# Attention into two expert layers on one core: key input loaded in stripes, with TensorE kept running at the start, and rows scattered by halves

## The chip, the cores and the metric

One core of one Trainium2 chip. The metric is the device time of one execution in microseconds (us), lower is better; most executions of one kernel agree within 0.3%.

## What is computed

Attention over pooled keys, then two mixture-of-experts layers of which each row takes one expert.

```python
B, N, C = q.shape                      # 2, 12288, 128
kv_pool = kv.reshape(B, H//4, 4, W//4, 4, C).mean(axis=(2, 4))   # H 384, W 32
k = v = kv_pool.reshape(B, -1, C) @ w_sr                         # 768 keys a batch
s = (q @ k.transpose(0, 2, 1)) / np.sqrt(C)
a = np.exp(s - s.max(-1, keepdims=True)); a /= a.sum(-1, keepdims=True) + 1e-9
x = (a @ v).reshape(B * N, D)
# layer 1 and layer 2 (8 experts, hidden width 1024), e = argmax of x @ w_gate:
out[mask] = gate_w[mask, None] * (np.maximum(x[mask] @ w1[e], 0) @ w2[e])
# layer 2 multiplies by sigmoid(x @ w_output_gate)[:, e] as well
```

## The kernel before

The queries come in 96 blocks of 256 rows (`NBLK`), four blocks to an iteration and two to a group of 512 rows. Each engine has a program of its own, in an order written out by hand; semaphores tie them together.

**Keys.** Of each batch, 768 keys are six chunks of 128. `load_kv` (L658) brings a chunk with four DMAs of 256 KB: partition p holds the 4x4 pixels of key p, and each DMA fetches one of the four image rows, 2 KB a partition. For the first batch VectorE adds the 16 pixels in one reduction (`kv_sum`, L1474), TensorE turns the result (L1040), ScalarE scales it (L1318), TensorE multiplies by `w_sr` (L1044, L1045), ScalarE and VectorE split the product into a high and a low part (`kv_high` L1323, `kv_low` L1480). For the second batch GpSimd adds in four steps (L884) in place, and TensorE turns and projects a chunk in two steps inside `turn_q` (L1058 for the turn, L1062 and L1063 for the projection) of blocks 4 to 15, a chunk every two blocks.

**Blocks.** `turn_q` (L1066) turns the queries of block c, four blocks ahead; `score` (L1079) multiplies them by all keys in three products; VectorE takes the maximum (L1503), ScalarE the exponential (L1349), TensorE turns the probabilities (L1103), multiplies them by the values (L1119) and by the gate matrix (`turn_rows`, L1138). ScalarE writes those rows to `rows` (L1373), two buffers that the groups use in turn. The lead (`lead`) fills this pipeline before the loop: `turn_q` of blocks 0 to 3 and `score` of blocks 0 and 1.

**Queries.** Each group of queries is one DMA of 256 KB on SyncE's queue (L647) into one of two buffers. Group 2 (blocks 4 and 5) and group 3 (blocks 6 and 7) are issued at the head of the first iteration, behind all key loads of both batches and the first four raw weight loads (L678, L683).

**Scatter.** When the places of a group's rows are known (`place`, L362), GpSimd issues four indirect DMAs (L390), 128 rows each, to the expert's bucket in HBM. In the loop of the queries it then splits expert weights (L903, L905). A buffer of `rows` may be written again when all four DMAs of its group have landed: ScalarE waits for that in `rows_out` (L1373), VectorE in `tile_rows_out` (L1632) of layer 1, whose rows go to `y_bucket` in the same way. The tiles of both layers are 256 rows; `up` is L1203, `down` L1220, the rows' gate product L1235. A tile's expert weights come from `w_table` in loads of 1 MB.

The waits that the change touches:

```python
# load_kv, L657        sp.wait_ge(kv_summed, c + 1)            second batch
# turn_q, L1057        pe.wait_ge(kv_fold, FOLDS * (late - KC + 1))
# rows_out, L1372      wait(act, r1.scattered[g], i, 64, 64 * (c // 4))
# tile_rows_out, L1624 if c % 2 == 0: wait(dve, r2.scattered[g], i, 64, 64 * (c // 4))
```

## Time and profile before

| | |
|---|---|
| median of 3 runs (lowest, highest) | 1969.69 us (1968.4, 1975.17) |
| profiled execution, its own time | 1974.21 us |
| its span | 1972.5 us |
| TensorE busy | 1906.3 us, 97% |
| VectorE, ScalarE, GpSimd busy | 1325.6, 1078.4, 743.9 us |
| DMA over the span | 94 GB/s; 244 GB/s in the first fortieth |

The profile gives busy time by engine, a chain of waits that ended last, groups of instructions with their mean duration and the idle time before them, and, for any stretch, each engine's busy time, the granted TensorE clock and what the DMA engines moved. TensorE is busy almost throughout, so the time can change only where it is idle or slow: the first 70 us, and a few places of some us.

### The profile page before, as it was taken

What the parts mean: (1) busy time and instruction counts of PE and PEld (TensorE: products, weight loads), DVE (VectorE), ACT (ScalarE), POOL (GpSimd) and SP (SyncE); (2) the same over time, 40 slices, a digit from 0 to 9 for tenths busy, and PEclk for the clock granted to TensorE, in tenths of its full rate; (3) what the DMA queues carried; (4) which work ended last, traced back from release to release, by engine and by line L of the source; (5) the groups of instructions that cost most, each with busy time, mean ns of one, the idle gap of its engine ahead of it and who ended that gap; (6) DMA issues with size and microseconds to landing.
All of it is one profiled execution on the core that took longest, in us unless ns stands there. A gap on an engine that the chain in (4) does not pass through costs nothing.

```text
span 1972.5 us, 53309 instructions
## 1 busy us (share of the span) xinstructions
PE 1906.3 (97%) x15870; PEld 1885.2 (96%) x15870; DVE 1325.6 (67%) x3505; ACT 1078.4 (55%) x2333; POOL 743.9 (38%) x821
## 2 busy tenths in 40 slices
PE   4799999999999899999999999999999999999998
PEld 3799999999999899999999999989999999999998
DVE  6577887777778576666666666756655555555554
ACT  2577777777777544444444444434454444444543
POOL 4456663366663232233223223323333333333333
PEclk9899999999999999999999999999999999999999
DMA  9355542145541321111241111141211114241111
GB/s 244 87 174 179 179 158 71 58 154 172 181 168 68 128 75 49 49 52 53 69 150 49 52 49 52 54 171 43 70 44 43 43 43 168 64 140 46 44 43 32
DMA packets 141496, 185.89 MB, mean 94 GB/s; under 512 B 17809, under 2 KB 95764, under 8 KB 137824
## 3 DMA queue, kind: packets, MB, share of 16 engines
q1 hardware_dynamic: 116096, 134.16, 22.5%
q0 software_dynamic: 25312, 50.65, 7.3%
q8 instruction: 44, 0.72, 0.1%
q14 instruction: 44, 0.36, 0.1%
HBM read 98.41 MB, written 87.63 MB: 94 GB/s over the span
## 4 chain that ended last, share of the span: by engine, by line
PE 92%; DMA 3%; SPq 2%; issue 1%; DVE 1%; POOL 0%; ACT 0%; POOLq 0%; DVEq 0%; ACTq 0%
PE psum L1203 28%; PE psum L1220 28%; PE psum L1119 10%; PE psum L1079 10%; PE psum L1103 6%; PE psum L1235 2%; PE psum L1138 2%; PE psum L1187 2%; SPq L658 1%; PE psum L1066 1%; PE psum L1237 1%; DMA w_split<-w_table 1%; DMA y_bucket<-kv_store,place 1%; DMA kv_store<-in_kv 1%; DMA q_in<-in_q 1%
## 5 line engine op out<-in xcount | busy, mean ns | idle before, releaser
L1614 DVE SCALAR_TENSOR_TENSOR h_lo<-psum,h_hi 128x512 fp32r<-128x512 f32 x800 | 553.0, 691 | 413.6 <-ACT h_hi L1410 411.5
L1410 ACT ACTIVATE h_hi<-psum 128x512 fp32r<-128x512 f32 x800 | 478.6, 598 | 638.2 <-PE psum L1203 635.3
L1203 PE MATMUL psum<-x_hi,w 128*128 128x256 f32 x1600 | 375.7, 297 | 5.4 <-issue 3.0
L390 POOL DMA_INDIRECT y_bucket<-kv_store,place x200 | 195.9, 979 | 474.5 <-DVE place L362 425.7
L1203 PE MATMUL psum<-x_hi,w_split 128*128 128x256 f32 x1600 | 365.6, 291 | 7.8 <-DMA w_split<-w_table 3.9
L1220 PE MATMUL psum<-h_hi,w 128*128 128x256 f32 x1600 | 354.4, 284 | 1.7 <-DVE h_lo L1614 1.7
L951 POOL DMA_INDIRECT out<-rows x200 | 194.6, 973 | 407.1 <-DVE rows L1634 369.3
L390 POOL DMA_INDIRECT x_bucket<-rows,place x192 | 189.7, 988 | 310.2 <-DVE place L362 264.3
L1203 PEld LDWEIGHTS psum<-x_hi,w 128*128 128x128 f32 x1600 | 277.8, 191 | 6.2 <-issue 5.2
L1203 PEld LDWEIGHTS psum<-x_hi,w_split 128*128 128x128 f32 x1600 | 273.5, 189 | 9.0 <-issue 9.0
L1220 PEld LDWEIGHTS psum<-h_hi,w 128*128 128x128 f32 x1600 | 279.0, 192 | 2.2 <-DVE h_lo L1614 2.2
L1509 DVE TENSOR_TENSOR pT_lo<-psum,pT_hi 128x512 fp32r<-128x512 f32 x288 | 198.4, 689 | 94.1 <-ACT pT_hi L1358 87.2
L1358 ACT ACTIVATE pT_hi<-psum 128x512 fp32r<-128x512 f32 x288 | 172.5, 599 | 116.4 <-PE psum L1103 115.8
L1220 PE MATMUL psum<-h_lo,w 128*128 128x256 f32 x800 | 227.0, 284 | 0.0
L1203 PE MATMUL psum<-x_lo,w 128*128 128x256 f32 x800 | 226.8, 283 | 0.0
L1203 PE MATMUL psum<-x_lo,w_split 128*128 128x256 f32 x800 | 224.8, 281 | 0.0
L1503 DVE TENSOR_REDUCE neg_max<-psum 128x1 f32<-128x768 f32 x192 | 182.8, 952 | 34.3 <-PE psum L1079 34.3
L1119 PE MATMUL psum<-pT_hi,kv_hi 128*128 128x256 f32 x576 | 185.6, 322 | 0.4 <-DVE pT_lo L1509 0.3
L1103 PE MATMUL psum<-ident,probs 128*128 128x128 f32 x1152 | 174.7, 274 | 1.2 <-DVE kv_lo L1480 1.1
L1220 PE MATMUL psum<-h_hi,kv_hi 128*128 128x256 f32 x800 | 174.3, 281 | 0.0
L1220 PE MATMUL psum<-h_hi,kv_lo 128*128 128x256 f32 x800 | 174.3, 280 | 0.0
L1349 ACT ACTIVATE probs<-psum,neg_max 128x768 f32<-128x768 f32 x192 | 172.2, 897 | 3.7 <-DVE neg_max L1503 3.7
(174 smaller groups left out, 4190.7 us busy)
## 6 DMA issues: line engine op xcount, KB each, us to landing
w_table<-w_split SPq DMA_DIRECT2D x64, 512.0 KB, 3.8
w_raw<-in_moe_w SPq DMA_DIRECT2D x64, 256.0 KB, 4.6
xr<-x_bucket SPq DMA_DIRECT2D x100, 132.0 KB, 2.5
xr<-y_bucket SPq DMA_DIRECT2D x100, 132.0 KB, 2.6
kv_store<-in_kv SPq DMA_DIRECT2D x48, 256.0 KB, 12.2
q_in<-in_q SPq DMA_DIRECT2D x48, 256.0 KB, 2.8
w<-w_table SPq DMA_DIRECT2D x12, 1024.0 KB, 5.3
w_split<-w_table SPq DMA_DIRECT2D x8, 1024.0 KB, 6.6
```

The source lines that it names most:

```text
L390: nc.gpsimd.indirect_dma_start(r.bucket[:, :], bass.IndirectOffsetOnAxis(r.place[:, g, s:s + 1], 0), r.rows[:, g, s, LG:], None, bounds_ch ...
L951: nc.gpsimd.indirect_dma_start(out[:, :], bass.IndirectOffsetOnAxis(rows[:, g, s, LG + ID:LG + ID + 1].bitcast(I32), 0), rows[:, g, s, LG: ...
L1079: ins = nc.tensor.matmul(bank[2 * s + m][:, 0:SPLIT], a[:, c % 2, s * P:(s + 1) * P], b[:, keys, 0, :], start=n == 0, stop=n == 2)
L1103: ins = nc.tensor.transpose(ps[:, m * BLOCK + s * P:m * BLOCK + (s + 1) * P], probs[:, c % 2, s, (2 * j + m) * P:(2 * j + m + 1) * P], ide ...
L1119: ins = nc.tensor.matmul(o_bank[:, 0:BLOCK], a[:, key, 1, :], b[:, j, at], start=j == m == n == 0, stop=j == PAIRS - 1 and m == 1 and n == 2)
L1203: ins = nc.tensor.matmul(bank[p][:, m * BLOCK:(m + 1) * BLOCK], layer.w1[c % 2][:, hl, f], x[:, c % 2, :], start=k == 0, stop=k == 2)
L1220: ins = nc.tensor.matmul(bank[4][:, 0:BLOCK], layer.w2[c % 2][:, hl, 2 * p + m, :], h[:, p, t], start=p == m == k == 0, stop=p == HP - 1 a ...
L1358: nc.scalar.activation(pT_hi[:, j, :], bank[4 + j % 2][:, :], ACT.Copy) \
L1410: nc.scalar.activation(h_hi[:, p, :], bank[p][:, :], ACT.Relu).then_inc(h_hi_done, 1)
L1503: nc.vector.tensor_reduce(neg_max[:, c % 2, s:s + 1], scores_ps(s), AX.XY, ALU.max, negate=True).then_inc(maxed, 1)
L1509: nc.vector.tensor_tensor(pT_lo[:, j, :], bank[4 + j % 2][:, :], pT_hi[:, j, :].bitcast(F32), ALU.subtract).then_inc(p_lo_done, 1)
L1614: nc.vector.scalar_tensor_tensor(h_lo[:, p, :], bank[p][:, :], 0.0, h_hi[:, p, :].bitcast(F32), ALU.max, ALU.subtract).then_inc(h_lo_done, 1)
```

## The change

Four things.

1. **Stripes.** The key input of a batch comes as 12 stripes of 16 image rows, one DMA of 512 KB each, 4 KB a partition; partition p holds eight neighbouring pixels of one image row. VectorE (first batch) and GpSimd (second batch) add in two steps only along the row. TensorE does the rest: `pool_keys` multiplies the partial sums by `key_of`, a 0/1 matrix of 128x32 that adds the four image rows of a key and turns the result in one product. The loads of the second batch wait for that product (`kv_turned`).
2. **The order of loads.** Query group 0 goes behind the sixth stripe, group 1 behind the twelfth, group 2 behind the fourth stripe of the second batch; group 3 stays where it was, behind all keys and the raw weights.
3. **TensorE at work.** 14 products of ones (bank 3, never read) before the first chunk and 1 + 4 within each; `turn_q` of blocks 0 and 1 and the first half of block 0's scores go between the chunks. GpSimd makes `ones` and `ident` first, and begins its sums when VectorE has done all of its own.
4. **Scatter by halves.** Each group's four indirect DMAs are two halves, one for each block, with semaphores of their own. The second half waits further: in the query loop for the turned probabilities of block 2g+5, elsewhere for the second `up` of tile 2g+5. `rows_out` and `tile_rows_out` wait only for their own block's half.

```diff
-                def load_kv(n):
+                def load_kv(b, k):
...
                     if b:
-                        sp.wait_ge(kv_summed, c + 1)
-                    for k in range(POOL):
-                        sp.dma_start(kv_in[:, c, k, :], src[k]).then_inc(kv_loaded[c], 16)
+                        sp.wait_ge(kv_turned, k // 2 + 1)
+                    sp.dma_start(kv_in[:, k].rearrange("p a j c -> p (a j c)"),
+                                 kv[b, k * STRIPE:(k + 1) * STRIPE].rearrange("h (w r) c -> (h w) (r c)", r=RUN)) \
+                        .then_inc(kv_loaded[k], 16)
...
+                pool.wait_ge(kv_summed, STRIPES)
+                for k in range(STRIPES):
+                    pool.wait_ge(kv_loaded[k], 32)
+                    pool.tensor_tensor(kv_in[:, k, :, 0:2, :], kv_in[:, k, :, 0:2, :], kv_in[:, k, :, 2:4, :],
+                                       ALU.add).then_inc(kv_fold, 1)
+                    pool.wait_ge(kv_fold, FOLDS * k + 1)
+                    pool.tensor_tensor(kv_in[:, k, :, 0, :], kv_in[:, k, :, 0, :], kv_in[:, k, :, 1, :],
+                                       ALU.add).then_inc(kv_fold, 1)
...
+                def warm(count):
+                    for _ in range(count):
+                        nc.tensor.matmul(bank[3][:, :], ones[:, :], bcast_mid(ones[:, :], 4), start=True, stop=True)
+                def pool_keys(n, ps, first=False):
+                    for k in (2 * n, 2 * n + 1):
+                        if first:
+                            pe.wait_ge(kv_summed, k + 1)
+                        for a in range(2):
+                            at = ((k % 2) * 2 + a) * (P // 4)
+                            ins = nc.tensor.matmul(ps[:, at:at + P // 4], kv_in[:, k, a, 0, :],
+                                                   key_of[:, :, :].rearrange("p h w -> p (h w)"), start=True, stop=True)
+                    ins.then_inc(kv_turned, 1)
...
-        def scatter(pool, r, i, gc):
+        def scatter(pool, r, i, gc, h):
...
-                wait(pool, r.place_done, i, 2, gc + 1)
+                if h == 0:
+                    wait(pool, r.place_done, i, 2, gc + 1)
+                elif r.n == 1 and live(i, 2 * gc + 5, NBLK, UNROLL):
+                    wait(pool, p_turned, i, PAIRS * UNROLL, PAIRS * (2 * gc + 5) + 2)
+                else:
+                    wait(pool, up_done, i - NIT if r.n == 1 else i, HP * UNROLL, HP * (2 * gc + 5) + 2)
...
-                        wait(act, r1.scattered[g], i, 64, 64 * (c // 4))
+                        wait(act, r1.scattered[g][c % 2], i, 32, 32 * (c // 4))
...
-                            if c % 2 == 0:
-                                wait(dve, r2.scattered[g], i, 64, 64 * (c // 4))
+                            if not at(i, c, TILES - 1):
+                                wait(dve, r2.scattered[g][c % 2], i, 32, 32 * (c // 4))
```

How the order moves, at three places. SyncE's queue from its start, before (names: `in_kv` the key input, `in_q` the queries, `in_moe_w` the raw weights):

```order
L658 DMA kv_store<-in_kv 128x1x512 x12
L647 DMA q_in<-in_q 128x512
L658 DMA kv_store<-in_kv 128x1x512 [waits kv_summed]
L658 DMA kv_store<-in_kv 128x1x512 x3
L678 DMA w_raw<-in_moe_w 128x512 x2
L683 DMA w_raw<-in_moe_w 128x4x128 x2
L647 DMA q_in<-in_q 128x512 [waits q_turned] x4
```

and now:

```order
L665 DMA kv_store<-in_kv 128x1024 x6
L659 DMA q_in<-in_q 128x512
L665 DMA kv_store<-in_kv 128x1024 [waits kv_turned] x4
L659 DMA q_in<-in_q 128x512 [waits q_turned]
L665 DMA kv_store<-in_kv 128x1024 [waits kv_turned] x8
L691 DMA w_raw<-in_moe_w 128x512 x2
L696 DMA w_raw<-in_moe_w 128x4x128 x2
L659 DMA q_in<-in_q 128x512 [waits q_turned] x3
```

One query load has left the four behind the raw weights and stands between the stripes of the second batch; the three that remain begin with group 3.

TensorE, from one chunk of keys to the next (the third chunk of the first batch), before:

```order
L1040 MATMUL psum<-ident,pooled 128x128 [waits kv_scaled,kv_summed]
L1044 MATMUL psum<-pooledT,wsr 128x128 [waits kv_lo_done,kv_scaled]
L1045 MATMUL psum<-wsr,pooledT 128x128
L1066 MATMUL psum<-ident,q_in 128x128 [waits q_lo_done,q_loaded0]
L1079 MATMUL psum<-kv_hi,q_hi 128x384 [waits q_lo_done,const_in,kv_lo_done]
```

and now:

```order
L1081 MATMUL psum<-key_of,kv_store 128x32 [waits kv_summed,kv_scaled]
L1081 MATMUL psum<-key_of,kv_store 128x32
L1081 MATMUL psum<-key_of,kv_store 128x32 [waits kv_summed]
L1072 MATMUL psum<-ones 128x512
L1088 MATMUL psum<-pooledT,wsr 128x128 [waits kv_scaled,kv_lo_done]
L1089 MATMUL psum<-wsr,pooledT 128x128
L1106 MATMUL psum<-ident,q_in 128x128 [waits q_loaded0,const_pool]
L1072 MATMUL psum<-ones 128x512 x4
```

The turn of queries stands inside the chunk, and products of ones fill what was a wait.

GpSimd in the first iteration of the query loop, group 0 (`rows` the rows to scatter, `place` where to), before:

```order
L390 DMA x_bucket<-rows,place 262400x192 [waits ids_done,place_done1]
L390 DMA x_bucket<-rows,place 262400x192 x3
L903 CAST w_split<-w_raw 128x512 [waits raw_in0_0]
L905 TENSOR_TENSOR w_split<-w_raw,w_split 128x512 [waits split_done0]
L903 CAST w_split<-w_raw 128x512 [waits raw_in0_1]
```

and now:

```order
L398 DMA x_bucket<-rows,place 262400x192 [waits ids_done,place_done1]
L398 DMA x_bucket<-rows,place 262400x192
L922 CAST w_split<-w_raw 128x512 [waits raw_in0_0]
L924 TENSOR_TENSOR w_split<-w_raw,w_split 128x512 [waits split_done0]
L398 DMA x_bucket<-rows,place 262400x192 [waits p_turned]
L922 CAST w_split<-w_raw 128x512 [waits raw_in0_1]
```

Two of the four indirect DMAs have moved behind a weight split and a wait of their own.

## Rows read from the trace of the kernel before

**Rows 1.** TensorE's waits: who, for whom, us in total, times, longest.
```profile
PE psum L1040 <- DVE pooled L1474: 23.8, 6, 11.4
PE psum L1058 <- DMA q_in<-in_q: 11.5, 1, 11.5
...
PE psum L277 <- ACT rows L1373: 3.2, 1, 3.2
...
PE psum L1220 <- DVE h_lo L1614: 1.7, 2, 1.5
```
**Rows 2.** Timeline of the lead: start us, us, what [idle before, releaser].
```profile
30.40 3.58 DVE L1474 TENSOR_REDUCE pooled<-kv_store 128x128 f32<-128x2048 f32 x1 [1.30 <-DMA kv_store<-in_kv]
...
37.87 0.67 PE L1079 MATMUL psum<-kv_hi,q_hi 128*128 128x384 f32 x1
...
38.33 0.52 PE L1079 MATMUL psum<-kv_lo,q_hi 128*128 128x384 f32 x1
...
43.08 0.34 PE L1079 MATMUL psum<-kv_lo,q_hi 128*128 128x384 f32 x1
```
**Rows 3.** The chain of waits, 61 to 83 us: start us, us, what.
```profile
61.21 0.47 PE psum L1058
...
69.44 0.22 PE psum L1062 x2
...
82.43 0.22 PE psum L1062 x2
```
**Rows 4.** Stretches: length, busy by engine, granted clock, DMA share, GB/s.
```profile
60.00:70.00 10.00, 8.79 (x56) 8.76 (x57) 4.33 (x8) 4.50 (x10) 4.79 (x5) 0.76 0.01 5
```
**Rows 5.** Stretches with full DMA queues, the same columns.
```profile
18.00:22.00 4.00, 1.06 (x3) 0.76 (x4) 3.75 (x3) 0.46 (x2) 0.00 (x0) 1.00 1.06 252
...
54.00:58.00 4.00, 0.00 (x0) 0.00 (x0) 0.00 (x0) 0.00 (x0) 3.84 (x4) 0.57 1.08 289
...
1732.00:1736.00 4.00, 1.81 (x16) 1.60 (x15) 1.14 (x4) 0.54 (x2) 1.23 (x2) 1.00 1.02 390
```
**Rows 6.** The page's groups: VectorE's sum of 512 columns, xcount | busy, mean ns.
```profile
L1509 DVE TENSOR_TENSOR pT_lo<-psum,pT_hi 128x512 fp32r<-128x512 f32 x288 | 198.4, 689 | 94.1 <-ACT pT_hi L1358 87.2
```
**Rows 7.** Instructions writing kv_store: ns min/median/max, first and last start, forms.
```profile
L884 POOL TENSOR_TENSOR kv_store<-kv_store x18: 723/1272/2394, 34.5 to 63.6; 128x1024 f32<-128x1024 f32 x6, 128x512 f32<-128x512 f32 x6, 128x256 f32<-128x256 f32 x6
```
**Rows 8.** Timeline of a plain stretch of the query loop.
```profile
206.41 1.01 POOL L390 DMA_INDIRECT x_bucket<-rows,place  x1 [3.63 <-DVE place L362]
...
207.27 0.39 ACT L1373 ACTIVATE rows<-psum 128x272 f32<-128x272 f32 x1
...
209.64 0.60 PE L1103 MATMUL psum<-ident,probs 128*128 128x128 f32 x4
```
**Rows 9.** DMA to landing of the scatters (L390), us min/median/max.
```profile
DMA to landing us min/median/max: 2.3/2.3/3.6
```
**Rows 10.** Timeline at the end of the queries.
```profile
661.60 0.99 POOL L390 DMA_INDIRECT x_bucket<-rows,place  x1 [6.49 <-DVE place L362]
...
671.67 0.40 ACT L1373 ACTIVATE rows<-psum 128x272 f32<-128x272 f32 x1 [5.62 <-DMA x_bucket<-rows,place]
```
**Rows 11.** The chain of waits, the same place.
```profile
665.45 6.13 DMA x_bucket<-rows,place
```
**Rows 12.** Timeline of layer 1, before layer 2's first weights.
```profile
1289.37 0.97 POOL L390 DMA_INDIRECT y_bucket<-kv_store,place  x1 [8.51 <-DVE place L362]
...
1300.52 0.17 DVE L1632 COPY kv_store<-xr 128x2 int32<-128x2 int32 x1 [5.46 <-DMA y_bucket<-kv_store,place]
```
**Rows 13.** The same stretch, TensorE.
```profile
1294.04 0.65 PE L1235 MATMUL psum<-gates,oT 128*128 128x144 f32 x4
...
1302.52 0.65 PE L1235 MATMUL psum<-gates,oT 128*128 128x144 f32 x4
...
1311.45 0.66 PE L1235 MATMUL psum<-gates,oT 128*128 128x144 f32 x4
```
**Rows 14.** VectorE's waits.
```profile
DVE kv_store L1632 <- DMA y_bucket<-kv_store,place: 43.5, 47, 5.5
```

More of the change, by code:

```diff
@@ L696, in iteration @@
                     for h in range(2):
-                        if live(i, 2 + h, NGRP, 2):
+                        if live(i, 2 + h, NGRP, 2) and not (isinstance(i, int) and i == h == 0):
                             load_q(i, 2 + h)
@@ L839, in _, with diagonal @@
             def _(pool):
-                eyes = (ident, gates[0][:, E:], gates[1][:, 2 * E:])
+                def diagonal(eye):
+                    return pool.affine_select(out=eye[:, :], in_=eye[:, :], compare_op=ALU.not_equal, fill=1.0, base=0,
+                                              pattern=[[-1, P]], channel_multiplier=1)
+                pool.memset(ones[:, :], 1.0).then_inc(ones_done, 1)
+                pool.memset(ident[:, :], 0.0).then_inc(const_pool, 1)
+                pool.wait_ge(const_pool, 1)
+                diagonal(ident).then_inc(ident_done, 1)
+                eyes = (gates[0][:, E:], gates[1][:, 2 * E:])
                 for eye in eyes:
@@ L912, in iteration @@
                             split(n, item, 2 * gc)
+                        scatter(pool, r1, i, gc, 1)
+                        if item is not None:
                             split(n, item, 2 * gc + 1)
@@ L920, in _ @@
                         iteration(i, n, i - n * HALF)
-                    with pool.Fori(n * HALF + E, (n + 1) * HALF) as i:
+                    with pool.Fori(n * HALF + E, (n + 1) * HALF - n) as i:
                         iteration(i, n, None)
+                iteration(NIT - 1, 1, None)
                 for g in range(2):
-                    pool.wait_ge(r1.scattered[g], 64 * NGRP // 2)
+                    for h in range(2):
+                        pool.wait_ge(r1.scattered[g][h], 32 * NGRP // 2)
                 pool.sem_inc(r1.all_out, 1)
@@ L928, in _ @@
                     for gc in range(2):
-                        scatter(pool, r2, i, gc)
+                        for h in range(2):
+                            scatter(pool, r2, i, gc, h)
                 last = layers[1].last(pool, plan1)
@@ L1068, in turn_q, with score @@
                     ins.then_inc(q_turned, 1)
-                def score(i, c, s, batch):
+                def score(i, c, s, batch, halves=(0, 1)):
                     if not live(i, c, NBLK, UNROLL):
@@ L1075, in score @@
                     wait(pe, probs_done, i, 2 * UNROLL, 2 * (c - 1) + s + 1)
-                    for m in range(2):
+                    for m in halves:
                         keys = slice(batch * KC + m * (KC // 2), batch * KC + (m + 1) * (KC // 2))
@@ L1376, in lead @@
                 def lead():
-                    q_high(0, 0)
-                    q_high(0, 1)
+                    for n in range(KC):
+                        kv_scale(n, first_keys(n))
+                        kv_high(n, first_kv(n))
+                        if n in (2, 3):
+                            q_high(0, n - 2)
                     exps(0, 0, 0)
@@ L1526, in lead @@
                 def lead():
-                    q_low(0, 0)
-                    q_low(0, 1)
+                    kv_sum(0)
+                    for n in range(KC):
+                        if n + 1 < KC:
+                            kv_sum(n + 1)
+                        kv_low(n, first_kv(n))
+                        if n in (2, 3):
+                            q_low(0, n - 2)
                     maxima(0, 0, 0)
```

177 lines of the change are left out of this document (95 added, 82 removed).

## The prediction

> **What bounds the kernel now.** I read TensorE's waits first, since that engine is busy almost throughout and only its idle or slow stretches can be won. There are two kinds [rows 1]: 23.8 us of waiting for VectorE's sums of keys and 11.5 us for one query load, both in the first 70 us, and single waits of 1 to 3 us far later, behind `rows` and `h_lo`. Everything between runs back to back, so a microsecond taken from the lead is a microsecond off the end.
>
> The timeline of the lead [rows 2] shows what stands behind the sums. The last reduction of the first batch begins at 30.40, having waited for the key load, and lasts 3.58; the first score product starts at 37.87 and its successor takes 0.52 us, where the same product takes 0.34 us later. So the load bounds the start, and TensorE begins slowly. In the chain [rows 3] TensorE reaches `turn_q` of block 4 at 61.21, after the 11.5 us wait, that is it was ready at 49.7; block 5 follows at 69.44, block 7 at 82.43. Two blocks in the steady state take 13.0, the first after the wait 8.2, so 1.7 us went to the slow clock: the granted clock of 60 to 70 us is 0.76 [rows 4], after TensorE had stood idle.
>
> The stretches with full DMA queues [rows 5] give the rates. Key loads, 2 KB a partition: 252 GB/s at a DMA share of 1.06. Near the end of the lead, where query and raw weight loads follow, 289 GB/s, also in 2 KB pieces or smaller. Expert weights, 8 KB a partition: 390 GB/s. The lead is bound by bytes in a queue.
>
> **The change, part by part.** *Rate of the stripes.* A key piece is now 4 KB. Over 16 engines a 2 KB piece takes 16 x 2048 B / 252 GB/s = 130 ns and an 8 KB piece 336 ns; between them in proportion, 4 KB take 199 ns, 329 GB/s. The bounds are 252 and 390; I take 320, near the middle value but below it, since no row shows it. "DMA: Bandwidth & Descriptors" of the Trainium skill (Specifications) puts line rate at 512 B and more, so by it the pieces were long enough already and the rate would stay at 252. The rows at 252 and 390 speak against that; what it would give is the first rival.
>
> *The first batch.* Ahead of its last byte stand 6.29 MB of keys and about 0.6 MB of other loads and fills: 6.9 MB / 252 GB/s = 27.4 us, and the data was there at 30.4, so 3.0 us are latency. Now: 3.0 + 6.29/0.320 + 0.6/0.289 = 24.7 us. The sum behind it was one instruction of 3.58; it becomes two of 512 and 256 columns. A sum of 512 columns takes 0.69 [rows 6], the smaller about 0.4: 1.1 a stripe, against 1.6 between stripes, so VectorE keeps up. From the end of the last sum (33.98) to the first score (37.87) went 3.9 us, with the turn of block 1's queries in it, which is now done before, and with slow products; I take 2.6 (bounds 2 and 3.9). The scores of the second key half start at 24.7 + 1.1 + 2.6 = 28.4 instead of 37.87.
>
> *The products of ones* fill waits. A product of 384 columns takes 0.34 us from start to end [rows 2] and overlaps its neighbours, so one of 512 columns takes 0.25 to 0.45; I take 0.25, and five are 1.2 us of a chunk's 3.3. Only the last three stand before the scores, under the split of the last chunk by ScalarE and VectorE. If the clock does not rise they cost double, and the covered wait is gone; that is the third rival. From the first score to `turn_q` of block 4 was 49.7 - 37.9 = 11.8, of it about ten products 0.15 too late; half of block 0's scores are now done earlier too, but VectorE and ScalarE set that stretch. I take 10.3 (bounds 9.5 and 11.8): 38.7.
>
> *The query load.* Group 2 now stands before two thirds of the second batch and lands at about 33; that 11.5 us wait is gone. What is late next is group 3, still last in the queue, needed by block 6, two blocks or 13.0 us later: 38.7 + 13.0 = 51.7. It lands at 3.0 + 12.58/0.320 + 2.44/0.289 = 50.7, with all keys, four query loads, raw weights and fills ahead of or in it. So it just makes it, by 1 us. Before, block 6 was at 82.43 - 6.5 = 75.9. **The lead gives 75.9 - 51.7 = 24.2 us.** At 252 GB/s the load lands at 61.4 against a need of 57.0, a new wait of 4.4 and up to 1.7 of slow clock: gain 12.8 to 14.5. At 390 need bounds, at 48.2: gain 27.7.
>
> *GpSimd's sums* of the second batch take 1.27 + 0.72 = 2.0 a stripe [rows 7] and start behind VectorE's last at 25.8: the first chunk is ready at 30, for a need of 38.7, the sixth at 51, for a need some 60 us later. The 4.2 us a chunk against 13.0 make this free. SyncE's new wait for `kv_turned` holds up query group 2 and everything behind it, but each chunk is turned some 4 us after landing, and 12 stripes lie ahead of the waiting load: free.
>
> *The scatter, in the plain loop.* Places come at 206.41, `rows` is written at 207.27 and every 6.4 us, TensorE turns the second part of the probabilities at 209.64 [rows 8]. The first half is out after two issues of 1.3 us, by 209.0, and lands 2.3 later [rows 9], at 211.3, for a need at 213.6. A weight split of 1.9 us follows, then the second half: issued from 211.2, landed at 216.1, for a need at 220.0. No wait, no gain. One `up` of the next tile gates it likewise in layer 1.
>
> *At the end of the queries.* ScalarE waited 5.62 us for the four scatters [rows 10]: the last was issued at 665.45 and took 6.13 to land [rows 11], beside 1 MB weight loads. It needed its buffer at 666.05. Now two issues suffice: out at 663.9, landed at 666.2 (2.3) to 670.0 (6.1). Of 3.2 us idle TensorE and the slow clock after it, I take 3.5 us gained (0 to 5).
>
> *Before layer 2's weights.* VectorE waited 5.46 us to 1300.52 for scatters issued from 1289.37 on [rows 12]. Only the first two count now, landed at 1293.9 to 1297.7, needed at 1295.1. The rows' product stood at 1294.04, 1302.52, 1311.45 [rows 13]; a plain tile takes 6.45, so 2.0 + 2.5 us were lost, partly to slow clock. I take 4.0 (0 to 4.5). A smaller wait of the kind near 993 gives 0.5. Elsewhere VectorE's 47 waits, 0.9 each [rows 14], go but cost TensorE nothing.
>
> Sum: 24.2 + 3.5 + 4.0 + 0.5 = 32.2. The profiled execution took 1974.21, giving 1942.0; the median of the runs is 4.5 lower, 1969.69, giving **1937.5 us**.
>
> **The rivals.** *One: the stripes come no faster.* 289 GB/s in pieces of 2 KB show that piece length is not all; if something else holds the keys at 252, group 3 is the new wait, the lead gives 13.6, all 21.6: 1948. With the halves worth little besides, 1953. Against it: 390 GB/s with the same queue.
>
> *Two: the halves bring nothing.* If what delays a scatter beside a weight load is fixed, the first half lands as late as before; the chance is real since 6.13 was measured for the last one only. Then 24.7 gained: 1945.
>
> *Three: the products of ones do not raise the clock.* Then the change does not do what it says: scores again at 0.52, the chain longer, 1.5 + 1.3 us, and the work of a chunk nears its 3.3 us. 1940 to 1942.
>
> *Four, slower: the second half comes late for its buffer.* It is put behind a weight split and a wait; the slack is 3.9 us (220.0 against 216.1). If a raw weight load delays the split by more, ScalarE waits in each of 98 groups. From 4.2 us of delay on, 98 x 0.3 us eat the gain; at 4.4, 98 x 0.5 = 49 us against 32.2: 1986. Against it: raw weights are loaded an iteration ahead.
>
> **How the numbers follow.** Forecast 0.60, one 0.20, two 0.12, three 0.05, four 0.03. The range starts with 27.7 + 5 + 4.5 + 1 = 38 and a little more, 1930, and ends with rival one, 1954. A measurement of this kernel can tell about 0.3%, 6 us: faster is everything below 1963.8. All but rival four and an accident of the same size lie there: faster 0.94, the same 0.03, slower 0.03.
>
> **What would show it.** Right: 310 to 330 GB/s between 5 and 40 us; first scores near 28 at 0.34; TensorE waiting under 2 us for `q_in`, if at all for group 3; block 6 near 52; no wait of ScalarE over 3 us near 645, none of VectorE near 1270. Wrong: a rate near 252, with a wait of 4 us or more for group 3; repeated waits of ScalarE for scatters in the loop; a lead in which TensorE waits for its own chain instead of the stripes.

## The result and the profile after

| | before | after |
|---|---|---|
| median of the runs, us | 1972.37 (4 runs, 1968.4 to 1975.17) | 1942.97 (4 runs, 1941.76 to 1943.34) |
| profiled execution, us | 1974.21 | 1943.34 |
| span, us | 1972.5 | 1941.6 |
| TensorE busy | 1906.3 (97%) | 1911.5 (98%) |

The ratio of the changed kernel to the kernel before is 0.985, 95% interval 0.983 to 0.987: 29.4 us less, where most executions of one kernel agree within 0.3%. Forecast were 1937.5 us, in a range of 1930 to 1954, and faster. (The median before stood at 1969.69 over three runs; a fourth beside the changed kernel moved it to 1972.37.) The part on the change has one figure wrong: a stripe of 512 KB is 32 image rows, not 16.

TensorE's waits of the changed kernel (who, for whom, us in total, times, longest) answer to [rows 1]:

```profile
PE psum L1266 <- issue: 8.8, 2, 6.4
PE psum L1266 <- DMA w_split<-w_table: 2.9, 2, 1.7
PE psum L1081 <- DVE kv_store L1541: 2.1, 3, 1.1
PE psum L1119 <- ACT probs L1408: 1.8, 2, 1.4
```

The 23.8 us for sums have become 2.1, the 11.5 us for a query load have gone. What leads the list now is new: 8.8 us of "issue", time in which TensorE waited for nothing that the profile shows, 6.4 of it in one place.

Stretches of the changed kernel (length, busy by engine, granted clock, DMA share, GB/s) answer to [rows 5]:

```profile
12.00:36.00 24.00, 20.32 (x131) 16.50 (x130) 17.01 (x31) 9.40 (x24) 11.82 (x13) 1.00 1.03 405
...
36.00:40.00 4.00, 4.00 (x35) 4.00 (x34) 2.54 (x4) 2.69 (x8) 3.84 (x5) 1.00 1.09 363
40.00:44.00 4.00, 4.00 (x33) 3.96 (x33) 3.21 (x7) 2.84 (x6) 3.84 (x5) 1.00 0.30 88
```

With DMA shares as full as before, the queues move 405 GB/s in place of 252, and are done with the keys by 40 us. The timeline of the lead, in the columns of [rows 2]: the last sum on VectorE, GpSimd's first, the first score of the second key half, and the key products of blocks 4 and 6.

```profile
22.58 0.43 DVE L1541 TENSOR_TENSOR kv_store<-kv_store 128x256 f32<-128x256 f32 x1
...
23.71 1.26 POOL L898 TENSOR_TENSOR kv_store<-kv_store 128x512 f32<-128x512 f32 x1 [16.03 <-DMA kv_store<-in_kv]
...
26.22 0.45 PE L1119 MATMUL psum<-kv_hi,q_hi 128*128 128x384 f32 x1 [0.28 <-DVE kv_lo L1547]
...
36.40 0.97 PE L1081 MATMUL psum<-key_of,kv_store 128*128 128x32 f32 x8
...
50.05 0.97 PE L1081 MATMUL psum<-key_of,kv_store 128*128 128x32 f32 x8
```

The scores come 11.7 us earlier than in [rows 2], and block 6, which was worked out to start at 75.9 before, at 50.05. Behind the lead, the two places of [rows 10] and [rows 12]: ScalarE's waits for scatters at the end of the queries, and VectorE's copies before layer 2's weights.

```profile
635.05 0.40 ACT L1432 ACTIVATE rows<-psum 128x272 f32<-128x272 f32 x1 [0.47 <-DMA x_bucket<-rows,place]
...
640.67 0.40 ACT L1432 ACTIVATE rows<-psum 128x272 f32<-128x272 f32 x1 [0.85 <-DMA x_bucket<-rows,place]
...
1269.42 0.16 DVE L1698 COPY kv_store<-xr 128x2 int32<-128x2 int32 x1
...
1276.00 0.16 DVE L1698 COPY kv_store<-xr 128x2 int32<-128x2 int32 x1
```

5.62 us have become 0.47 and 0.85, and 5.46 nothing.

To see where the time went I set the two kernels side by side at ScalarE's `x_hi` of every expert tile (the tiles are 200, a plain one takes some 6.6 us in layer 1 and 6.1 in layer 2):

| tile | before, us | after, us | ahead by |
|---|---|---|---|
| 0 | 665.66 | 639.45 | 26.2 |
| 1 | 677.26 | 646.78 | 30.5 |
| 51 | 1010.16 | 977.96 | 32.2 |
| 96 | 1310.40 | 1274.00 | 36.4 |
| 196 | 1935.57 | 1898.35 | 37.2 |
| 197 | 1944.43 | 1913.52 | 30.9 |

So the lead gave 26.2, the end of the queries 4.3, the place near 1000 us 1.7, that before layer 2's weights 4.2 and small things 0.8. Between the tiles 196 and 197 6.3 of it were given back. There lies the 6.4 us wait; in the timeline of TensorE and of its weight loads (PEld) and in the stretch behind it:

```profile
1906.20 0.37 PE L1266 MATMUL psum<-x_hi,w_split 128*128 128x256 f32 x1 [6.38 <-issue]
...
1902.69 0.29 PEld L1266 LDWEIGHTS psum<-x_hi,w_split 128*128 128x128 f32 x1 [3.11 <-issue]
1906.20 0.29 PEld L1266 LDWEIGHTS psum<-x_lo,w_split 128*128 128x128 f32 x1 [3.22 <-issue]
...
1907.00:1911.00 4.00, 4.00 (x21) 4.00 (x20) 0.82 (x2) 1.19 (x2) 0.00 (x0) 0.50 0.02 4
```

There are two waits, one behind the other, at the first products behind the loop over layer 2's tiles; before, there was one at this place, 2.58 us on the product's row. The products behind it then run at a clock of 0.50, its lower level of 1.2 GHz, until about 1912, which they did not do before: 3.8 us more of waiting and some 2.5 us lost on slow products.

### The profile page after: what moved, and what is told of

Read it like the earlier page. It is cut to its first block and busy times, and to the rows that moved or that the text cites. A ratio compares the mean times of both kernels' runs of the same rounds, so it can differ in the third digit from the quotient of the medians.

```text
span 1941.6 us, 53830 instructions
## 1 busy us (share of the span) xinstructions
PE 1911.5 (98%) x15993; PEld 1888.5 (97%) x15993; DVE 1321.5 (68%) x3524; ACT 1077.4 (55%) x2333; POOL 739.1 (38%) x821
```

## The experiments

Three theories were to be told apart. Of the rate: the length of a partition's piece sets it (the prediction's), against the order of the addresses. Of the halves: the deferred second half, against the separate semaphores alone. Of the tail: where TensorE's program lies in memory, against something in the change's work. Beside them the products of ones were tried for what they are worth.

The twelve kernels ran in four groups, each on one chip together with the kernel before. The first group (`halves_only` to `pieces_apart`) ran where that takes 1970.39 us (13 runs). The others met chips on which the kernel before took 2219.43 (7 runs), 2139.97 (7) and 2243.88 us (11). There the layers' tiles are disturbed by many waits for issue of 1 to 2.5 us, which the first chip shows at a few places only; of such a run I read only the first 65 us and the exit of the last loop. `few_ones`' waits show what they are like:

```profile
PEld psum L1282 <- issue: 137.2, 121, 2.5
```

None of the kernels below leaves out a part of the computation; the products of ones feed no result.

### The halves without the lead

```diff
 (the kernel before, with the change's scatter in two halves alone)
-                        wait(act, r1.scattered[g], i, 64, 64 * (c // 4))
+                        wait(act, r1.scattered[g][c % 2], i, 32, 32 * (c // 4))
```

> The kernel before with the scatter halves alone: its key loads, query loads and lead are untouched. If the gains behind the lead belong to the halves (theory), tile 1 of layer 1 follows tile 0 by about 7.3 us instead of 11.6, the waits near 1000 us shrink by about 1.9 us and those near 1310 us by about 4.7 us, together 10 to 11 us, span near 1962. Rival: those places only moved because everything ran 26 us earlier against the weight loads; then under 3 us is gained. The lead gives 0 in either case. The wait of TensorE at tile 97 of layer 2 (2.6 us before, 6.4 after) is code loading: if it depends on the program's layout it may take any of these values here.

Measured: 1959.49 us (10 runs, 1955.44 to 1965.15), ratio 0.994 (0.993 to 0.996): 10.9 us less than before. Against the trace of before the tiles are ahead by 2.5 us at tile 0, 7.1 at tile 1, 10.0 at tile 51, 14.3 at tile 96 and 13.0 at tile 197. The first 2.5 come from the lead, which the edit does not touch and where 0 was expected; in this execution the query load is waited for less:

```profile
PE psum L1075 <- DMA q_in<-in_q: 9.5, 1, 9.5
```

It is 11.5 in [rows 1]. The rest is 4.6, 2.9 and 4.3 us at the three places that the prediction named. Rival two (the halves bring nothing) falls.

### The lead without the halves

All four scatters at once again, and their writers wait for all four.

```diff
-                for s in range(h * SUB, (h + 1) * SUB):
+                for s in range(GSUB):
...
-                        wait(act, r1.scattered[g][c % 2], i, 32, 32 * (c // 4))
+                        for half in range(2):
+                            wait(act, r1.scattered[g][half], i, 32, 32 * (c // 4))
```

> The changed kernel with the scatter as before: all four indirect DMAs at once, and whoever writes the buffer waits for all four. Theory: the lead keeps its 26 us, and the 10 to 11 us behind it are lost, so span 1941.6 + 10.8 = 1952 if tile 97 of layer 2 waits 6.4 us again, 1946 if it waits as before. Rival: the later waits do not return, since weight loads and scatters meet otherwise after an earlier start; span 1942 to 1944.

Measured: 1948.19 us (4 runs, 1945.15 to 1952.59), ratio 0.989 (0.986 to 0.993): 22.2 us less than before. Ahead by 25.7 us at tile 0, 29.7 at tile 1, 30.7 at tile 51 and 32.3 at tile 96. Even with the old waits the end of the queries loses less than before; ScalarE's wait there is

```profile
642.97 0.40 ACT L1429 ACTIVATE rows<-psum 128x272 f32<-128x272 f32 x1 [2.60 <-DMA x_bucket<-rows,place]
```

instead of the 5.62 of [rows 10]. VectorE's waits before layer 2's weights are back, 5.19 and 4.26 us. The only change to the end of the queries is that it comes earlier against the DMA queues; that scatters and weight loads meet otherwise is my reading of it, and wasn't tried by itself. The profiled execution is also the fastest of the four, 3.0 us under their median, so the tiles' figures are on the good side. The median lies between what theory (a span of 1952) and rival (1942 to 1944) expected: part of the gain that the prediction gave to the halves seems to come with the changed lead alone.

### Separate semaphores, no deferral

All four scatters are issued at once, but each half has its semaphore and each writer waits for its own.

```diff
-                if h == 0:
-                    wait(pool, r.place_done, i, 2, gc + 1)
-                elif r.n == 1 and live(i, 2 * gc + 5, NBLK, UNROLL):
...
-                for s in range(h * SUB, (h + 1) * SUB):
+                if h:
+                    return
+                wait(pool, r.place_done, i, 2, gc + 1)
+                pool.sem_inc(r.scatter_go, 1)
+                for s in range(GSUB):
```

> The changed kernel, with all four indirect DMAs issued at once, but each half still with a semaphore of its own and each writer waiting for its own half. If the separate semaphores alone bring the gain and the later issue of the second half brings none, this equals the changed kernel within 1 us up to tile 96 of layer 2. If holding the second half back matters (it lets the first land beside fewer bytes, and frees GpSimd for the weight split), 2 to 4 us are lost at the three places.

Measured: 1942.74 us (4 runs, 1941.43 to 1943.68), ratio 0.986 (0.982 to 0.989), the changed kernel's time. ScalarE's wait near 641 us is 0.87, as in the change, and VectorE's waits for scatters in layer 1 are 1.8 us in all, where the change has 2.3 and the kernel before 43.5 ([rows 14]). What the halves bring is that a writer no longer waits for the two scatters that don't read its half; holding the second pair back brings nothing that can be measured. Against `lead_only` it is 5.5 us.

### The length of the pieces

In two kernels each stripe comes by two DMAs of 256 KB with 2 KB a partition, as long as the pieces of the kernel before. In `pieces_apart` each takes every other 2 KB of the stripe; in `pieces_dense` each takes 16 whole image rows.

```diff
 pieces_apart
+                    src = kv[b, k * STRIPE:(k + 1) * STRIPE].rearrange("h (w a r) c -> a (h w) (r c)", a=2, r=POOL)
+                    for a in range(2):
+                        sp.dma_start(kv_in[:, k, a].rearrange("p j c -> p (j c)"), src[a]).then_inc(kv_loaded[k], 16)
 pieces_dense
+                    src = kv[b, k * STRIPE:(k + 1) * STRIPE].rearrange("(a h) (w r) c -> a (h w) (r c)", a=2, r=POOL)
```

> The changed kernel, but each stripe of keys is fetched by two DMAs of 256 KB: 2 KB a partition, every other 2 KB of the stripe. Theory of piece length: the key rate falls from about 400 GB/s to about 252, the lead becomes bound by loads, block 6 begins near 61 us instead of 50, span 1952 to 1954. Theory of address order (before, a DMA took 16 KB runs 64 KB apart): rate stays at 380 to 410, and span within 1 us of the changed kernel.

> The changed kernel, but each stripe of 32 image rows comes by two DMAs, each of 16 whole image rows (256 KB in one stretch of memory), 2 KB a partition; TensorE's 128x64 matrix of ones and zeros then picks 4-row groups of 4-pixel pieces. The maps come in the same order of addresses as with one DMA a stripe, in pieces of half the length. Theory A (what slowed the kernel before is the order of addresses: 16 engines each read 16 KB stretches 64 KB apart): keys still arrive at 380 to 410 GB/s between 12 and 36 us, span within 2 us of the changed kernel's 1941.6. Theory B (the length of a partition's piece decides): about 250 to 290 GB/s, block 6's scores some 10 us later, span about 1951. The chunks' last sums stay at 22.6 us by A, and come at about 30 us by B.

Measured: 1943.43 us and 2157.15 us (one run each, the second on a disturbed chip). The rates, in a stretch of `pieces_apart` and then of `pieces_dense`:

```profile
12.00:36.00 24.00, 20.55 (x120) 16.84 (x120) 16.02 (x31) 8.99 (x24) 10.95 (x11) 0.93 1.05 385
```

```profile
12.00:36.00 24.00, 20.20 (x130) 16.50 (x131) 17.18 (x31) 9.22 (x24) 10.94 (x11) 1.00 1.05 385
```

Both have 385 GB/s. With pieces of 2 KB the loads run at 95% of the change's rate, where the kernel before had 252 with 2 KB. The length of a piece is not what held it. (`pieces_apart` took the changed kernel's time, though its clock falls for a while near 32 us and its block 6 comes 1.6 us later. The matrix of `pieces_dense` is 128x32, not 128x64 as its expectation says.)

### The order of the addresses

The pieces stay at 4 KB and the DMA at 512 KB, but each takes every other pair of image rows out of 64: 16 stretches of 32 KB, which begin 64 KB apart. (In the kernel before they were 16 KB long, 64 KB apart.) TensorE adds two stripes in PSUM.

```diff
+                    src = kv[b, k // 2 * 2 * STRIPE:(k // 2 + 1) * 2 * STRIPE].rearrange(
+                        "(m j f) (w r) c -> j m (f w) (r c)", j=2, f=2, r=RUN)
+                    sp.dma_start(kv_in[:, k].rearrange("p a j c -> p (a j c)"), src[k % 2]).then_inc(kv_loaded[k], 16)
```

> The changed kernel, but each of the 512 KB DMAs takes every other pair of image rows out of 64: pieces of 4 KB a partition as in the change, 8 partitions reading one stretch of 32 KB, stretches 64 KB apart (that of the kernel before was 16 KB stretches 64 KB apart, in 2 KB pieces). TensorE folds two stripes into one sum in PSUM, so that a chunk's keys wait for both of its stripes. Theory A (address order decides): the rate between 12 and 36 us falls to between 250 and 330 GB/s, the last of the sums on VectorE comes at 26 to 30 us rather than at 22.6, and the span is 3 to 10 us longer than 1941.6. Theory B (length of a piece decides): 390 GB/s or more as in the change, the span within 1.5 us of it (half a microsecond of later keys aside).

Measured: 2162.95 us, one run on the disturbed chip of `pieces_dense`, 5.8 us more than that. The stretch, and TensorE at block 6:

```profile
12.00:36.00 24.00, 20.21 (x95) 13.44 (x93) 12.48 (x25) 4.23 (x13) 0.71 (x1) 0.74 1.04 246
```

```profile
65.08 1.51 PE L1081 MATMUL psum<-key_of,kv_store 128*128 128x64 f32 x8 [4.41 <-DMA q_in<-in_q]
```

246 GB/s: with the longer pieces the rate of the kernel before is back, under the expected 250 to 330, and VectorE's last sum begins at 32.6 us where 26 to 30 were expected. Block 6 waits 4.41 us for its queries, the new wait that rival one had described (4.4), and comes 15 us later than in the change. The order of the addresses decides: DMAs whose stretches begin 64 KB apart give 246 to 252 GB/s, DMAs that leave no gap or gaps of 2 KB give 385 to 405. The single packets in the traces say the same (medians between 12 and 28 us): one of 4 KB takes 161 ns in the change and 279 in `pitch_64k`, one of 2 KB 86 in both kernels with short pieces and 136 in the kernel before. The packets of a query group, whose 256 KB lie in one stretch, take 147 ns in `pitch_64k` between the others and 84 in the change, so what slows the others reaches a DMA whose own addresses lie close together.

The runs point the same way as a rule that the prediction overlooked. The Trainium skill, "DMA: Bandwidth & Descriptors", Latency and other measured facts, has copies slow down where the partitions' rows stand a large power of two apart: 207 GB/s at a pitch of 512 KiB, 164 at 2 MiB, 103 at 4 MiB. It has no figure for smaller pitches; here 64 KB between stretches cost 40%. Why it is so the runs don't settle, and the page calls its own reason an inference.

### The products of ones

Five kernels change their number: 14 at the start and 25 between the chunks are those of the change.

```diff
 few_ones: none between chunks (14 in all)
-                        warm(1)
...
-                            warm(4 if n < KC - 1 else 3)
+                            pass
 no_ones: none at all
-                    for _ in range(count):
+                    for _ in range(0):
 ones_16 and ones_10: 16 or 10 at the start
-                    warm(14)
+                    warm(16)
 half_ones: 2 in place of 4 and 3
-                            warm(4 if n < KC - 1 else 3)
+                            warm(2)
```

> The changed kernel without the products of ones between the six chunks (25 of 39; the 14 at the start stay). Theory A (from 16 us on the lead is bound by TensorE's own queue, three microseconds a chunk with some 1.5 of it in ones): the second-half scores come 1 to 2 us before 26.2 us, and the kernel gains 0.5 to 1.5 us. Theory B (the ones pay: without them TensorE idles in the gaps and its granted clock drops): the clock falls below full for a few microseconds between 12 and 36 us, products of 0.30 us take 0.5, and block 6 starts 1 to 3 us later than at 50.05. Beside it: the wait named issue at the first tile behind the last loop (6.4 us in the changed kernel, 2.6 before) lies where TensorE's program is entered by a jump; if it hangs on how the program is laid out in memory, it changes with the 25 instructions that are gone (3 or 6 us); if it hangs on something else in the change, it stays at 6.3 to 6.5.

> The changed kernel without any product of ones (all 39 gone; they feed no result). Rival three of the prediction, turned into a run: TensorE starts cold at about 10 us. Theory A (the ones hold the clock): the keys' projections and the first scores of 256 or 384 columns run at half rate (0.52 us instead of 0.3) until some microseconds after steady work begins, block 6's scores come 2 to 4 us later than 50.05, and the span is 2 to 4 us longer. Theory B (the clock rises by itself early enough, the ones are idle talk): within 1 us of the changed kernel, or faster. The issue wait behind the last loop as for the run before: 6.3 to 6.5 if the layout of the program plays no part, another value if it does.

> The changed kernel with 16 products of ones at the start instead of 14. The two more (0.33 us each, into a gap of 1.13 us in which TensorE waits for the first sum) cost the lead nothing; they put 4 instructions ahead of all the rest of TensorE's program. Theory A (the 6.4 us at the first tile behind the last loop are two fetches of the program one behind the other, 3.1 and 3.2 us on the weight loads' row, because the code that is jumped to ends a fetched piece there): a shift by 4 instructions moves the jump's target over that end, the wait is 2.6 to 3.2 us as before, and the kernel takes 1939 to 1940.5 us, 3 less. Theory B (the wait comes of something else in the change, or the place doesn't hang on so few instructions): 6.3 to 6.5 us again, and 1942 to 1944 us.

> The changed kernel with 10 products of ones at the start instead of 14: TensorE's program is 8 instructions shorter ahead of everything else, and idles 1.3 us longer before the first keys. Layout: by theory A of the run before, the target lies 8 instructions further ahead of the end of its piece; the second fetch is then met some 8 instructions (under a microsecond of work) later, so that the wait is still 5 to 6.5 us in two parts, with up to a microsecond of work between them, and the kernel stays at 1941 to 1944. Clock: if 10 are too few, the keys' projections take 0.6 to 0.77 us instead of 0.46 and block 6 starts 2 to 4 us late as without the ones between the chunks; if they do, nothing moves in the lead.

> The changed kernel with 2 products of ones instead of 4 (3 after the last) between chunks, those right behind the keys and at the start kept: 9 fewer in all, 18 instructions. Theory A (the lead from 16 us on is TensorE's own queue, of which the ones take their share; 3 ones a chunk are enough for the clock): the chunks' distance falls from 3.25 to about 2.8 us where sums no longer hold it, the second-half scores come 0.4 to 0.9 us before 26.2, and so does block 6. Theory B (each of them is needed): the granted clock falls below full between 12 and 36 us and block 6 starts 1 to 4 us after 50.05, as it did without them (54.5). The wait behind the last loop: one fetch (2.6 to 3.2 us), as with 25 and with 39 products fewer, or two (6.4), which tells how far the program must move.

Measured: `few_ones` 2137.28 (2134.64 to 2150.71), `no_ones` 2146.03 (2137.98 to 2160.57), ratios 0.966 (0.960 to 0.971) and 0.969 (0.962 to 0.976) on the second chip; `ones_16` 2056.67 (2048.6 to 2061.89), `ones_10` 2053.37 (2051.8 to 2059.64), `half_ones` 2054.99 (2041.94 to 2064.48), ratios 0.962 (0.958 to 0.966), 0.960 (0.956 to 0.963) and 0.960 (0.954 to 0.966) on the third; four runs each. On one chip the kernels can't be told apart by their times. The traces can:

| kernel | granted clock between 8 and 40 us | block 6's keys, us | waits at the last loop's exit, us |
|---|---|---|---|
| the change | 1.00 throughout | 50.05 | 3.11, 3.22 |
| `pieces_dense` (39 ones) | 1.00 throughout | 50.28 | 3.15, 3.27 |
| `few_ones` | below 1.00 in every 4 us, 0.50 from 12 to 24 and from 32 to 36 | 54.46 | 2.94 |
| `no_ones` | see below | 54.20 | 3.07 |
| `ones_16` | 0.57 and 0.58 from 16 to 24 | 53.46 | 3.13 |
| `ones_10` | 0.50 from 8 to 20, 0.81 from 20 to 24 | 54.78 | 3.34, then 2.64 later |
| `half_ones` | 1.00 throughout | 49.92 | 3.09, then 1.03 later |

In order, a stretch of `few_ones`, of `ones_16` and of `ones_10`:

```profile
16.00:20.00 4.00, 3.54 (x17) 3.44 (x17) 3.67 (x8) 1.05 (x3) 0.00 (x0) 0.50 1.02 409
```

```profile
16.00:20.00 4.00, 4.00 (x19) 3.01 (x18) 3.77 (x9) 0.67 (x2) 0.00 (x0) 0.57 1.02 409
```

```profile
12.00:16.00 4.00, 4.00 (x17) 2.91 (x16) 1.76 (x4) 0.66 (x2) 0.00 (x0) 0.50 1.03 416
```

The ones are worth 4.2 to 4.4 us of the lead (54.20 and 54.46 against 50.05; 3.9 to 4.2 against `pieces_dense` on the same chip), and the 14 at the start without the others give nothing. In `no_ones` the clock's column must be read with care:

```profile
16.00:20.00 4.00, 3.54 (x17) 3.44 (x17) 3.72 (x8) 1.04 (x3) 0.00 (x0) 1.00 1.03 410
```

```profile
15.66 0.77 PE L1088 MATMUL psum<-pooledT,wsr 128*128 128x128 f32 x2 [0.46 <-ACT pooledT L1381]
```

The column says 1.00, but the pair of products takes 0.77 us, as in `few_ones` at a clock of 0.50 and against 0.46 in the change. My reading is that TensorE had not been fast yet, and that the column shows only falls from full speed.

Which number holds the clock is not settled, with one trace of each. Nine fewer (`half_ones`) held it and brought block 6 only 0.13 us earlier, where 0.4 to 0.9 were expected of a lead bound by TensorE's queue: VectorE's last sum begins at 22.65 there and at 22.58 in the change, so TensorE's ones did not hold it up. Two more at the start, where I had expected nothing, lost the clock at 16 us and with it 3.4 us of the lead.

The exit of the last loop goes by the length of TensorE's program ahead of it. A product is two instructions (weight load and product), so `ones_16` moves the code by +4, `ones_10` by -8, `half_ones` by -18, `few_ones` by -50, `no_ones` by -78. The weight loads' waits of `ones_16`, then of `ones_10`, then of `half_ones`:

```profile
2012.41 0.19 PEld L1266 LDWEIGHTS psum<-x_hi,w_split 128*128 128x128 f32 x1 [3.13 <-issue]
```

```profile
2019.32 0.28 PEld L1266 LDWEIGHTS psum<-x_hi,w_split 128*128 128x128 f32 x1 [3.34 <-issue]
2023.10 0.29 PEld L1266 LDWEIGHTS psum<-x_hi,w_split 128*128 128x128 f32 x1 [2.64 <-issue]
```

```profile
2021.08 0.29 PEld L1266 LDWEIGHTS psum<-x_hi,w_split 128*128 128x128 f32 x1 [3.09 <-issue]
2024.32 0.29 PEld L1283 LDWEIGHTS psum<-h_lo,kv_lo 128*128 128x128 f32 x1 [1.03 <-issue]
```

With none moved, the second wait follows the first at once and is 3.22; 8 instructions away it comes after some work and is 2.64; 18 away 1.03; 50 and 78 away there is none; and with 4 more instructions ahead it is gone too, as if the place that is jumped to had passed the end of a piece. All five kernels whose TensorE lead is as long as the change's (`lead_only`, `own_sems`, `pieces_apart`, `pieces_dense`, `pitch_64k`) have 6.0 to 6.5 us on the product's row, and `halves_only`, with the old lead, 2.96. The pages of the change and of `ones_16` list the instruction packets:

```profile
q8 instruction: 46, 0.75, 0.2%
```

```profile
q8 instruction: 45, 0.74, 0.1%
```

In the change one of these packets starts at 1899.95 and one at 1903.73, 2.7 and 2.5 us before the two waits end. So the second wait of 3.2 us is the price of where the code came to lie, and of nothing that the change does. The slow clock behind it is so only in part. Of six traces with one wait here, four have the lower clock too (`half_split`, `no_ones`, `ones_16`, `halves_only`, waits of 2.78 to 2.96 us on the product's row) and two have not (the kernel before and `few_ones`, 2.58 and 2.73). In `halves_only`:

```profile
1924.00:1928.00 4.00, 4.00 (x19) 4.00 (x20) 0.69 (x1) 0.60 (x1) 0.94 (x1) 0.50 0.25 70
```

From tile 196 to 197 the six take 8.9 to 11.9 us, the six with the double wait 13.6 to 15.2 (the change 15.2, the kernel before 8.9). The Trainium skill, "Runtime: NRT & Kernel Launch", Instruction fetch mechanics, says that an engine's program is fetched in blocks of 16 KiB and that a taken branch out of the fetched window waits for its block. The trace agrees: the 46 packets of 0.75 MB together are 16 KB each. That the end of a block right behind the target costs a second wait is worked out from these runs.

### What the runs point to

Two ones between chunks, and 11 of the first 14 cut in two of half the columns, so that the program is 4 instructions longer than the change's for about the same work.

```diff
-                    warm(14)
+                    warm(3)
+                    warm(11, 2)
...
-                            warm(4 if n < KC - 1 else 3)
+                            warm(2)
```

> The version that the runs so far point to: the changed kernel with 2 products of ones between chunks instead of 4 (as in the run before with 9 fewer), and 11 of the 14 at the start cut into two of 256 columns each, so that TensorE's program is 4 instructions longer than the changed kernel's, as with 16 at the start, but works on ones for about as long (1.06 to 5.7 us). Theory A (layout decides the wait behind the last loop; two ones between chunks hold the clock): one fetch of 2.6 to 3.2 us at the last loop's end, the granted clock at 1.00 from 8 to 40 us, block 6's keys at 49.9 to 50.1 us; against the changed kernel 3 to 4 us less, that is 1939 to 1940 on a chip where that takes 1943 (ratio to the kernel before 0.983 to 0.984), and lost in the spread on a chip where the layers' tiles are disturbed. Theory B (clock in the lead by chance): the granted clock falls in some stretch between 12 and 36 us, and block 6's keys come 1 to 4 us later.

Measured: 2149.15 us (6 runs, 2145.64 to 2153.79), on a chip where the kernel before takes 2243.88; ratio 0.958 (0.954 to 0.963). In its trace, a stretch, block 6's keys, and the exit of the last loop:

```profile
16.00:20.00 4.00, 3.76 (x29) 3.08 (x27) 3.77 (x9) 1.59 (x5) 0.00 (x0) 1.00 1.02 409
```

```profile
49.74 0.53 PE L1082 MATMUL psum<-key_of,kv_store 128*128 128x32 f32 x4
...
2109.45 0.22 PEld L1268 LDWEIGHTS psum<-x_hi,w_split 128*128 128x128 f32 x1 [2.98 <-issue]
```

Both are about as theory A has it: the clock is full from 8 to 40 us, block 6 is 0.31 us earlier than in the change, and there is one fetch. That this makes 1939 us on the first chip was not measured; the changed kernel itself was not run on this one.

That the kernels with several runs have ratios of 0.958 to 0.969 on the three disturbed chips, against 0.985 for the change on its own, says that kernels with the changed lead and scatters take 73 to 95 us less than the one before there (the two with one run 56 and 62). I have no trace of the kernel before on such a chip and leave its cause open.

## Why the prediction was right

**The bound** was read rightly: the lead was bound by its loads, and the two waits of [rows 1] fell from 35.3 to 2.1 us.

**The rate** was too low, and its reason was wrong. The step "in proportion, 4 KB take 199 ns, 329 GB/s" took the difference between [rows 5]'s 252 and 390 for one of piece length. The measured 405 lies above the upper bound (391 over 5 to 40 us, where 310 to 330 were to show that the reading is right), and `pieces_apart`, `pieces_dense` and `pitch_64k` show that length is worth 5% and the addresses' order 40%. "The rows at 252 and 390 speak against that" was no argument against the rule of the Trainium skill ("DMA: Bandwidth & Descriptors", Specifications) that pieces of 512 B are long enough: pieces of 2 KB at 385 GB/s come within 5% of it, and rival one, which was hung on it, fell for another reason. A third row stood there and was used only as a rival's argument: 289 GB/s in pieces of 2 KB and less.

**The first batch** was in sooner: its last stripe landed at 21.4 us where 24.7 was forecast, 3.3 earlier, and the last sum ended at 23.0 against 25.8, 2.8 earlier. "So VectorE keeps up" held at the forecast rate and not quite at the real one. The sum of 1.1 a stripe left out that VectorE also splits keys and queries, 0.42 each. It last waits for a key load at 15.0 and works without a pause from 16.28 to 23.3, 2.8 to 3.0 us a chunk with both splits, where two stripes come every 2.6:

```profile
16.00:20.00 4.00, 3.73 (x26) 2.58 (x24) 3.77 (x9) 1.59 (x5) 0.00 (x0) 1.00 1.02 407
```

```profile
16.28 0.69 DVE L1538 TENSOR_TENSOR kv_store<-kv_store 128x512 f32<-128x512 f32 x1
...
21.86 0.68 DVE L1538 TENSOR_TENSOR kv_store<-kv_store 128x512 f32<-128x512 f32 x1
```

Second-half scores came at 26.22 for a forecast of 28.4: another 0.6 was given back between the sums and the scores (3.2 for 2.6), where TensorE first finishes block 0's first half of scores.

**From there to block 6**: 10.2 us to block 4 where 10.3 was taken, and 13.65 for two blocks where 13.0 was taken from [rows 3], since GpSimd's keys bring eight small products. Block 6 at 50.05 for 51.7, no wait for group 3 (landed at 42.9, not 50.7) or any other query load. The lead gave 25.9 by this row and 26.2 at tile 0, for 24.2: right in kind, 2 us too small. Luck had a part in this. With the landing as it was, the prediction's own steps lead to its other sum, block 6 at 48.2 and a gain of 27.7; the rate made the landing 3.3 us too late, and the steps behind it were some 1.7 too short, so that half of the first error was hidden.

**GpSimd's sums** were free as forecast: they start at 23.71, take 1.26 and 0.73 a stripe and are done at 48.4, and no engine waits for them.

**The ones**: rival three had them fail to raise the clock, at a price of 2.8 us and more. They raised it, and `no_ones` sets that price at 4.2.

**The halves**: 4.3 for 3.5 at the end of the queries, 1.7 for 0.5 near 1000, 4.2 for 4.0 before layer 2's weights. Sizes were near, and "now two issues suffice" is what `own_sems` shows: the gain is in the semaphores, and the later issue of the second half brings nothing. What the prediction didn't see is that either change alone brings much of this: of the 10.2 us between tiles 0 and 96 6.6 came with the changed lead alone in `lead_only`'s one trace, while `halves_only` has 11.8 there. Rival four, the second half late for its buffer, did not come up: ScalarE has no repeated wait for scatters in the loop.

**What the sum lacked** is the term at the end: -6.3 us at the exit of the last loop. Without it the profiled execution would have been 1937.0, where the sum said 1942.0; with it, 1943.34. So the nearness of the forecast is two errors of opposite sign, gains 5.0 us larger than forecast (37.2 for 32.2) and a loss of 6.3 us of which no step spoke. The measured median lies 5.5 us above the predicted one, and 2.7 of these are the median before, which with its fourth run is that much higher than the one the sum went by.

## What to carry to other kernels

When two loads have different rates, compare the order of their addresses before the length of the pieces: DMAs over one stretch of memory (or every other 2 KB of it) ran at 385 to 405 GB/s and those whose stretches stood 64 KB apart at 246 to 252, in pieces of 2 KB or 4 KB alike. When a load gets faster, add up all that its consumer does in the same time: VectorE's sums fitted between two stripes, its sums and splits together did not. Give each writer its own semaphore for the transfers that it really waits for before reordering the transfers. After any edit that changes a program's length, look at the issue waits behind loops and branches: a jump to just ahead of the end of a fetched block cost two fetches here, 6.4 us, and a shift by four instructions took one of them away.

## What the runs showed of the hardware

- One fetch behind a jump took 2.6 to 3.6 us on the weight loads' row, two in a row 5.96 to 6.53 on the product's row. Behind idle times of 6.0 to 6.5 us products ran at 0.50 of granted clock for 2.7 to 5.8 us, in all six traces; behind 2.58 and 2.73 us they did not, in one trace each, and behind 2.78 to 2.96 in four they did. These are too few to draw a limit from.
- The granted clock's column reads 1.00 for a TensorE that is still slow from its start; durations (0.77 for 0.46 us) tell it.
- Filling work holds the clock in no simple way: with 39 ones it was full in four traces and fell to 0.75 and 0.83 from 28 to 36 us in a fifth (`pieces_apart`, whose block 6 came at 51.66; `pitch_64k`, where TensorE waits for slower loads, lost it too), 41 (two more at the start) lost it for 8 us, 30 held it.
- On three of the four chips of the experiments the kernel before took 9 to 14% longer than on the first.
